# Seven products, then six mixing tiles: another order of work in a mixture-of-experts stage

## The chip, the cores and the metric

The kernel runs on one core of one Trainium2 chip. The core has TensorE (PE in the views; its weight loads are shown apart as PEld), VectorE (DVE), ScalarE (ACT), GpSimd (POOL) and SyncE (SP), which run their own instruction streams and meet only at semaphores. The metric is the device time of one execution in microseconds (us).

## The reference, cut to what matters

Local attention with a few global positions makes x (1536 tokens, 512 wide). Then follow a mixture of experts and a gated layer:

```python
def _moe_ref(x, domain_probs, w1, w2):
    p = domain_probs / (domain_probs.sum(-1, keepdims=True) + 1e-09)
    out = np.zeros((N, D))
    for e in range(E):                       # 4 experts, hidden width 1024
        h = np.maximum(x @ w1[e], 0.0)
        out += p[:, e:e + 1] * (h @ w2[e])
    return out

def _moe2_ref(x, w_in, w_out, g_ln):
    h = x @ w_in
    ...                                      # softmax gate, layer norm
    return ln @ w_out
```

## The kernel before

**Steps.** The experts are worked in 32 steps, numbered s = 0 to 31. A step takes a group of 256 hidden columns (16 groups g) for one half of the tokens. Every fp32 operand is split in a high and a low part, and each product of two matrices is three matmuls (high by high, high by low, low by high). x @ w1 is done as a 2 by 2 block product with seven products in place of eight (Strassen-Winograd), in the order 1, 2, 6, 7, 5, 4, 3: `product(s, n)`, six matmuls of 128x384 each, 42 in a step. h @ w2 is done in six token tiles: `mix(s, t)`, six matmuls of 128x512 each, 36 in a step. TensorE mixes step s-1 while it makes the products of step s. Steps 4 to 27 are a hardware loop of four steps a turn; the others are written out.

**What follows the products.** The seven products share four PSUM banks and the mixing tiles three. ScalarE copies product 1 to `kept` (`keep`, L1211). VectorE adds up the products in seven additions that count `p_sum`: `first_block`, `second_sum`, `third_sum`, `last_block`, `fourth_sum`, `lower_block`, `right_block` (L1549 to L1577). Each reads a PSUM bank. Four of them finish a block of h. ScalarE then writes relu of that block as the high part (`relu_hi`, L1216) and VectorE the low part (`relu_lo`, L1582, both inputs in SBUF, counts `h_split`). `add_up(s, t)` (L1598) adds a mixed tile times its expert weight to `acc` and frees the tile's PSUM bank.

**Waits of TensorE that matter here.** Product 5 waits for `keep`, product 4 for `first_block`, product 3 for `second_sum` of its own step, since they reuse the banks; mix t of a step waits for `add_up` t-3.

**GpSimd** prepares the weights with operations that read and write SBUF alone: `weigh_sums` and `weigh_parts` split a group of w1 and start when all products of step 2g-3 are there; `split_w2` starts when all tiles of step 2g-3 are mixed. After the last group, SyncE loads w_in, and GpSimd makes four block sums of it (128x1024 each, L770 to L777, once w_in is there and the products of step 29 are) and then seven low parts (`win_lo_at`, L783, each after ScalarE's high part `win_hi_part`, L1356). ScalarE's order in steps 30 and 31 is written out by hand.

**The tail** (from L1028 and L1104 on) turns `acc`, multiplies by w_in and w_out and writes the output.

Of the kernel before, what the change touches and what calls it, by code (L numbers as in the profile page):

```python
# [23 lines left out]
START = 16  # L24
# [29 lines left out]
def attention_experts_solu_kernel(nc, H, qkW, qT, kT, v, counts_in, probs, w1, w2, w_in, w_out, gain, out):  # L54
# [16 lines left out]
    TILES = QB  # L71
# [31 lines left out]
    with ExitStack() as base:  # L103
# [740 lines left out]
        def _(pe):  # L844

            def product(s, n, i, g, slot, bt):

                bank = p_bank(i, n)
                if n == 1:
                    pe.wait_ge(w1_ready, g + 1)  # L850
                    at_least(pe, p_sum, SETS * s - 4)
                if n == 2:
                    at_least(pe, p_sum, SETS * s - 2)
                if n == 6:
                    at_least(pe, p_sum, SETS * s - 1)
                if n == 7:
                    at_least(pe, p_sum, SETS * s)
                if n == 5:
                    pe.wait_ge(p_kept, s + 1)
                if n == 4:  # L860
                    pe.wait_ge(p_sum, SETS * s + 1)
                if n == 3:
                    pe.wait_ge(p_sum, SETS * s + 2)
                part = {1: 0, 2: 1, 4: 2, 3: 3, 5: 4, 6: 5, 7: 6}[n]
                for kk in range(2):
                    for w, x in ((1, 1), (1, 0), (0, 1)):
                        mm = nc.tensor.matmul(bank, ws[slot][:, w, part, kk, :], xs[:, 2 * bt + kk, x, part, :],  # L867
                                              start=(kk == 0 and w == 1 and x == 1),
                                              stop=(kk == 1 and w == 0))
                mm.then_inc(p_done, 1)  # L870

            def mix(s, t, slot, ring, g):

                if t == 0:
                    pe.wait_ge(w2_ready, g + 1)
                    pe.wait_ge(h_split, BLOCKS * s + 3)
                if t == 3:
                    pe.wait_ge(h_split, BLOCKS * s + BLOCKS)
                if isinstance(s, int) and s == LAST and t == 5:
                    pe.wait_ge(x2_raw, 6)  # L880
                else:
                    at_least(pe, acc_written, TILES * s + t + 1 - Y_BANKS + (isinstance(s, int) and s == LAST and t == 4))
                tok = slice((t % 3) * P, (t % 3 + 1) * P)
                for f in range(2):
                    b = 2 * f + t // 3
                    for h, w in ((1, 1), (1, 0), (0, 1)):
                        mm = nc.tensor.matmul(mixed_at(s, t), hs[ring][:, h, b, tok], w2s[slot][:, w, f, :],  # L887
                                              start=(f == 0 and h == 1 and w == 1), stop=(f == 1 and h == 0))
                mm.then_inc(y_done, 1)
# [128 lines left out]
            def turn_x(s):  # L1018
# [9 lines left out]
                    mm = nc.tensor.transpose(turned_at(s)[:, k * P:(k + 1) * P], acc[:, s, k * P:(k + 1) * P], ident[:, :])  # L1028
                mm.then_inc(x_final, 1)

            def step(a, i):

                s, g, last = 4 * a + i, group(a, i), 4 * a + i - 1
                slot, bt, ring = slot_of(a, i), batch(a, i), (i - 1) % 2
                last_slot, last_g = (slot_of(a, i - 1), group(a, i - 1)) if i else (1, 2 * a - 1)
                new = isinstance(a, int) and s == 1
                if new:
                    pe.wait_ge(xs_sum, START + 21)
                product(s, 1, i, g, slot, bt)
                product(s, 2, i, g, slot, bt)  # L1040
                mix(last, 0, last_slot, ring, last_g)
                mix(last, 1, last_slot, ring, last_g)
                if new:
                    pe.wait_ge(xs_sum, START + 24)
                mix(last, 2, last_slot, ring, last_g)
                if new:
                    pe.wait_ge(xs_lo, START + 13)
                product(s, 6, i, g, slot, bt)
                if new:
                    pe.wait_ge(xs_lo, START + 14)  # L1050
                product(s, 7, i, g, slot, bt)
                mix(last, 3, last_slot, ring, last_g)
                if new:
                    pe.wait_ge(xs_lo, START + 15)
                product(s, 5, i, g, slot, bt)
                mix(last, 4, last_slot, ring, last_g)
                if new:
                    pe.wait_ge(xs_lo, START + 16)
                product(s, 4, i, g, slot, bt)
                if isinstance(a, int) and s == LAST:  # L1060
                    turn_x(0)
                    turn_x(1)
                product(s, 3, i, g, slot, bt)
                mix(last, 5, last_slot, ring, last_g)

            for i in range(1, 4):
                step(0, i)
# [126 lines left out]
        def _(act):  # L1194
# [12 lines left out]
            def keep(s, i):  # L1207

                act.wait_ge(p_done, SETS * s + 1)
                at_least(act, p_sum, SETS * s - 5)  # L1210
                nc.scalar.activation(kept[:, 0, :], p_bank(i, 1), ACT.Copy).then_inc(p_kept, 1)  # L1211

            def relu_hi(s, b, bt):

                act.wait_ge(p_sum, SETS * s + {0: 1, 3: 4, 2: 6, 1: 7}[b])
                nc.scalar.activation(hs[bt][:, 1, b], hs_sum[bt][:, 0, b], ACT.Relu).then_inc(hhi_ready, 1)  # L1216
# [151 lines left out]
                for c in chunks:  # L1368
                    wout_hi_part(c)

            keep(LAST - 1, 2)
            relu_hi(LAST - 1, 0, 0)
            act.wait_ge(win_loaded, 16)
            act.wait_ge(p_done, SETS * (LAST - 1))
            for at in range(3):
# [126 lines left out]
        def _(dve):  # L1502
# [294 lines left out]
            with dve.Else():  # L1797
                attend_wide()

            def halve(a, i):  # L1800

                s, bt = 4 * a + i, i % 2
                first = isinstance(a, int) and s <= 2
                expert = a // 2 if i else (a - 1) // 2
                last_bt = batch(a, i - 1) if i else 1
                first_block(s, i)
                add_up(s - 1, 0, last_bt, expert, first)
                relu_lo(s, 0, bt)
                add_up(s - 1, 1, last_bt, expert, first)
                add_up(s - 1, 2, last_bt, expert, first)  # L1810
                second_sum(s, i)
                third_sum(s, i)
                add_up(s - 1, 3, last_bt, expert, first)
                last_block(s, i)
                fourth_sum(s, i)
                add_up(s - 1, 4, last_bt, expert, first)
                relu_lo(s, 3, bt)
                lower_block(s, i)
                right_block(s, i)
                relu_lo(s, 2, bt)  # L1820
                relu_lo(s, 1, bt)
                add_up(s - 1, 5, last_bt, expert, first)

            for i in range(1, 4):
                halve(0, i)
# [224 lines left out]
```

## Time and profile before

| what | value |
|---|---|
| median of 3 runs | 741.29 us (740.76 to 741.61) |
| the profiled execution's own time | 741.24 us |
| its span in the trace | 739.2 us |
| PE busy | 734.8 us (99% of the span) |
| DVE, ACT, POOL busy | 516.6, 223.5, 348.1 us |
| granted clock of TensorE | full speed in all 40 slices |

The time of an execution is about 2 us more than its span. Busy PE is pipelined matmuls, so that a start-to-start distance tells more than a busy time: a 128x512 matmul is shown as 0.39 us long, but the next one starts after 0.23 us.

### The profile page before, as it was taken

To read this page: it belongs to the slowest core of one execution; us is meant where nothing else is said; L and a number is where in the kernel's file an instruction comes from. 1 tells how busy PE (TensorE), PEld (TensorE's weight loads), DVE (VectorE), ACT (ScalarE), POOL (GpSimd) and SP (SyncE) were. 2 spreads that over 40 slices of the span, in tenths; PEclk is the share of its full clock that TensorE was granted. 3 is DMA by queue.
4 is the path that set the end of the run, shared out by engine and by line. 5 is a ranking of instruction groups with operands and counts; after the bars stand their busy time and mean duration, and the time that the engine had idled before them with its cause. 6 is when DMAs were issued, how large, how long until landed. Compare 5 with 4: busy or idle time off the path is not lost.

```text
span 739.2 us, 12549 instructions
## 1 busy us (share of the span) xinstructions
PE 734.8 (99%) x3992; PEld 650.0 (88%) x3992; DVE 516.6 (70%) x1031; ACT 223.5 (30%) x421; POOL 348.1 (47%) x336
## 2 busy tenths in 40 slices
PE   9999999999999999999999999999999999999998
PEld 7888899999898998899998989989998888888887
DVE  5777767676666766767666676766668858767773
ACT  5667741111111121111111111111115466433332
POOL 4558446253542536435264351644519986432400
PEclk9999999999999999999999999999999999999999
DMA  8835300100101000010000101000030300000001
GB/s 227 241 109 147 106 31 1 58 29 30 33 25 57 28 28 28 28 57 28 28 28 28 57 8 48 28 28 0 0 114 5 110 1 11 19 30 28 15 30 43
DMA packets 38226, 36.11 MB, mean 49 GB/s; under 512 B 14512, under 2 KB 31152, under 8 KB 38192
## 3 DMA queue, kind: packets, MB, share of 16 engines
q1 hardware_dynamic: 36448, 33.46, 14.3%
q10 hardware_dynamic: 1744, 2.23, 0.9%
q8 instruction: 17, 0.28, 0.2%
q14 instruction: 17, 0.14, 0.1%
HBM read 32.54 MB, written 3.15 MB: 48 GB/s over the span
## 4 chain that ended last, share of the span: by engine, by line
PE 97%; DVE 2%; DMA 1%; issue 0%; SPq 0%; ACT 0%; POOL 0%; DVEq 0%
PE y_ps L887 35%; PE p_ps L867 32%; PE o_ps L934 5%; PE pT_ps L915 3%; PE s_ps L905 3%; PE up_ps L1106 3%; PE up_ps L1104 3%; PE up_ps L1105 3%; PE out_ps L1134 2%; PE out_ps L1136 2%; PE out_ps L1135 2%; PE lnT_ps L1119 1%; PE xt_ps L945 1%; PE xr_ps L1028 1%; DMA qk<-in_qkW 1%
## 5 line engine op out<-in xcount | busy, mean ns | idle before, releaser
L887 PE MATMUL y_ps<-w2s,hs 128*128 128x512 f32 x1140 | 283.0, 393 | 0.2 <-DVE acc L1598 0.2
L867 PE MATMUL p_ps<-xs,ws 128*128 128x384 f32 x1344 | 254.9, 335 | 0.0
L867 PEld LDWEIGHTS p_ps<-xs,ws 128*128 128x128 f32 x1344 | 237.5, 188 | 10.7
L887 PEld LDWEIGHTS y_ps<-w2s,hs 128*128 128x128 f32 x1140 | 211.8, 188 | 38.9 <-DVE acc L1598 0.8
L1598 DVE SCALAR_TENSOR_TENSOR acc<-y_ps,pr,acc 128x512 f32<-128x512 f32 x178 | 132.9, 748 | 77.0 <-PE y_ps L887 76.3
L1216 ACT ACTIVATE hs<-hs_sum 128x384 fp32r<-128x384 f32 x128 | 67.2, 525 | 350.2 <-DVE hs_sum L1563 231.6
L1582 DVE SCALAR_TENSOR_TENSOR hs<-hs_sum,hs 128x384 fp32r<-128x384 f32 x128 | 97.4, 771 | 4.3 <-ACT hs L1216 2.3
L648 POOL TENSOR_TENSOR ws_sum<-raw_sum 128x256 f32<-128x256 f32 x16 | 11.8, 741 | 148.8 <-PE p_ps L867 144.6
L679 POOL CAST w2s<-raw_sum 128x1024 fp32r<-128x1024 f32 x16 | 16.9, 1056 | 84.9 <-PE y_ps L887 84.9
L1229 ACT ACTIVATE neg_s<-neg_s,row 128x256 f32<-128x256 f32 (+1 forms) x96 | 41.9, 482 | 27.1 <-DVE row L1620 26.9
L1620 DVE CUSTOM_DVE_ANT_0 neg_s<-s_ps,bias 128x256 f32<-128x256 f32 (+1 forms) x87 | 31.2, 398 | 15.9 <-PE s_ps L905 13.2
L934 PE MATMUL o_ps<-v_sb,pT 128*128 128x65 f32 x352 | 42.3, 272 | 0.0
L934 PEld LDWEIGHTS o_ps<-v_sb,pT 128*128 128x128 f32 x352 | 41.2, 192 | 0.7 <-DVE x_pair L1646 0.7
L682 POOL TENSOR_TENSOR w2s<-raw_sum,w2s 128x1024 fp32r<-128x1024 f32 x16 | 38.4, 2400 | 2.9 <-POOL w2s L679 2.9
L671 POOL TENSOR_TENSOR ws<-ws_sum,ws 128x1024 fp32r<-128x1024 f32 x16 | 38.4, 2398 | 2.9 <-POOL ws L668 2.9
L824 POOL TENSOR_TENSOR stats<-stats,minus_half 128x1 f32<-128x1 f32 x12 | 10.3, 854 | 59.0 <-DVE stats L1918 59.0
L1549 DVE TENSOR_TENSOR hs_sum<-p_ps,kept 128x384 f32<-128x384 f32 x32 | 17.8, 557 | 26.7 <-PE p_ps L867 26.4
L1104 PE MATMUL up_ps<-win_hi,x 128*128 128x512 f32 x84 | 34.1, 406 | 0.0
L1106 PE MATMUL up_ps<-win_hi,x 128*128 128x512 f32 x84 | 32.9, 392 | 0.0
L1135 PE MATMUL out_ps<-wout_lo_a,ln_hi 128*128 128x512 f32 x77 | 30.0, 389 | 0.0
L1211 ACT ACTIVATE kept<-p_ps 128x384 f32<-128x384 f32 x32 | 15.8, 492 | 42.0 <-PE p_ps L867 42.0
L1558 DVE TENSOR_TENSOR kept<-p_ps,kept 128x384 f32<-128x384 f32 x32 | 17.8, 557 | 13.9 <-PE p_ps L867 13.5
(200 smaller groups left out, 976.0 us busy)
## 6 DMA issues: line engine op xcount, KB each, us to landing
raw_sum<-in_w SPq DMA_DIRECT2D x28, 512.0 KB, 3.3
qk<-in_qkW SPq DMA_DIRECT2D x16, 256.0 KB, 3.3
qk<-in_qkW SPq DMA_DIRECT2D x31, 128.0 KB, 3.4
v_sb<-in_v SPq DMA_DIRECT2D x16, 192.0 KB, 3.2
out<-o_sb SPq DMA_DIRECT2D x11, 256.0 KB, 2.0
raw_sum<-in_w ACTq DMA_DIRECT2D x4, 512.0 KB, 6.6
raw_sum<-in_w_in SPq DMA_DIRECT2D x1, 2048.0 KB, 7.6
wout_lo_a_sum<-in_w_out SPq DMA_DIRECT2D x1, 1792.0 KB, 7.6
```

The lines of the kernel that those rows point to most:

```text
L671: nc.gpsimd.tensor_tensor(lo[:, 3:7], sum_[:, 3:7], f32(hi[:, 3:7]), ALU.subtract).then_inc(w1_ready, 1)
L682: nc.gpsimd.tensor_tensor(lo, rows, f32(hi), ALU.subtract).then_inc(w2_ready, 1)
L867: mm = nc.tensor.matmul(bank, ws[slot][:, w, part, kk, :], xs[:, 2 * bt + kk, x, part, :], start=(kk == 0 and w == 1 and x == 1), stop=(kk ...
L887: mm = nc.tensor.matmul(mixed_at(s, t), hs[ring][:, h, b, tok], w2s[slot][:, w, f, :], start=(f == 0 and h == 1 and w == 1), stop=(f == 1 ...
L934: mm = nc.tensor.matmul(o_ps[:, m, i * DV:(i + 1) * DV], pT[c % 2][:, e, (2 * m + half) * P:(2 * m + half + 1) * P], v_sb[:, p, m, at, :], ...
L1104: nc.tensor.matmul(up_bank(q, n), x_hi, win_hi[:, part, kk], start=(kk == 0), stop=False)
L1106: mm = nc.tensor.matmul(up_bank(q, n), x_lo, win_hi[:, part, kk], start=False, stop=(kk == KH - 1))
L1135: nc.tensor.matmul(out_ps[m][:, :], ln_hi[m][:, c, :], wout_lo(c), start=False, stop=False)
L1216: nc.scalar.activation(hs[bt][:, 1, b], hs_sum[bt][:, 0, b], ACT.Relu).then_inc(hhi_ready, 1)
L1229: nc.scalar.activation(tile, tile, ACT.Exp, bias=row[:, b // STEPS_PAIR, m, i:i + 1], scale=-1.0).then_inc(exp_ready, 1)
L1582: nc.vector.scalar_tensor_tensor(hs[bt][:, 0, b], hs_sum[bt][:, 0, b], 0.0, f32(hs[bt][:, 1, b]), ALU.max, ALU.subtract).then_inc(h_split, 1)
L1598: nc.vector.scalar_tensor_tensor(acc[:, tile, :], mixed_at(s, t), weight, acc[:, tile, :], ALU.mult, ALU.add).then_inc(acc_written, 1)
```

## The change

TensorE's `step` now makes all seven products of the step and then mixes all six tiles of the last step. Step 1, whose products wait for the attention stage, keeps the old order in a function of its own (`first_step`; the waits for `xs_sum` and `xs_lo` are only there). VectorE's `halve` follows: the additions and low parts come first, `add_up` of tile 0 is put before the low part of block 1, and the other five `add_up` come after it; step 1 keeps its order (`first_halve`). ScalarE makes the first five high parts of w_in before it starts step 30, and the last two before the `relu_hi` of block 3. No instruction is added or removed.

```diff
             def step(a, i):
...
                 if new:
                     pe.wait_ge(xs_sum, START + 21)
+                    first_step(s, i, g, slot, bt, ring, last, last_slot, last_g)
+                    return
                 product(s, 1, i, g, slot, bt)
                 product(s, 2, i, g, slot, bt)
-                mix(last, 0, last_slot, ring, last_g)
-                mix(last, 1, last_slot, ring, last_g)
...
-                mix(last, 2, last_slot, ring, last_g)
...
                 product(s, 6, i, g, slot, bt)
...
                 product(s, 7, i, g, slot, bt)
-                mix(last, 3, last_slot, ring, last_g)
...
                 product(s, 5, i, g, slot, bt)
-                mix(last, 4, last_slot, ring, last_g)
...
                 product(s, 4, i, g, slot, bt)
                 if isinstance(a, int) and s == LAST:
                     turn_x(0)
                     turn_x(1)
                 product(s, 3, i, g, slot, bt)
-                mix(last, 5, last_slot, ring, last_g)
+                for t in range(TILES):
+                    mix(last, t, last_slot, ring, last_g)
...
-            keep(LAST - 1, 2)
-            relu_hi(LAST - 1, 0, 0)
             act.wait_ge(win_loaded, 16)
             act.wait_ge(p_done, SETS * (LAST - 1))
             for at in range(3):
...
             for at in range(3, 5):
                 win_hi_part(at)
-            relu_hi(LAST - 1, 3, 0)
+            keep(LAST - 1, 2)
+            relu_hi(LAST - 1, 0, 0)
             act.wait_ge(win_sum, 4)
             for at in range(5, SETS):
                 win_hi_part(at)
+            relu_hi(LAST - 1, 3, 0)
             relu_hi(LAST - 1, 2, 0)
             relu_hi(LAST - 1, 1, 0)
...
+                first_block(s, i)
+                relu_lo(s, 0, bt)
+                second_sum(s, i)
+                third_sum(s, i)
+                last_block(s, i)
+                fourth_sum(s, i)
+                relu_lo(s, 3, bt)
+                lower_block(s, i)
+                right_block(s, i)
+                relu_lo(s, 2, bt)
+                add_up(s - 1, 0, last_bt, expert, first)
+                relu_lo(s, 1, bt)
+                for t in range(1, TILES):
+                    add_up(s - 1, t, last_bt, expert, first)
```

TensorE, one of the steps 28 to 30, before (L867 is a product's matmul, L887 a mixing tile's):

```order
L867 MATMUL p_ps<-xs,ws 128x384 x12
L887 MATMUL y_ps<-w2s,hs 128x512 x18
L867 MATMUL p_ps<-xs,ws 128x384 x12
L887 MATMUL y_ps<-w2s,hs 128x512 x6
L867 MATMUL p_ps<-xs,ws 128x384 x6
L887 MATMUL y_ps<-w2s,hs 128x512 x6
L867 MATMUL p_ps<-xs,ws 128x384 x12
L887 MATMUL y_ps<-w2s,hs 128x512 x6
```

and steps 28 to 30 with the change:

```order
L867 MATMUL p_ps<-xs,ws 128x384 x42
L887 MATMUL y_ps<-w2s,hs 128x512 x36
L867 MATMUL p_ps<-xs,ws 128x384 x42
L887 MATMUL y_ps<-w2s,hs 128x512 x36
L867 MATMUL p_ps<-xs,ws 128x384 x42
L887 MATMUL y_ps<-w2s,hs 128x512 x36
```

Eight changes between the two kinds of matmul in a step have become two.

VectorE, the start of step 30 before (L1549 is `first_block`, L1598 `add_up`, L1582 `relu_lo`):

```order
L1549 TENSOR_TENSOR hs0_sum<-p_ps3,kept 128x384
L1598 SCALAR_TENSOR_TENSOR acc<-y_ps0,pr,acc 128x512
L1582 SCALAR_TENSOR_TENSOR hs0<-hs0_sum,hs0 128x384
L1598 SCALAR_TENSOR_TENSOR acc<-y_ps1,pr,acc 128x512
L1598 SCALAR_TENSOR_TENSOR acc<-y_ps2,pr,acc 128x512
L1553 TENSOR_TENSOR kept<-p_ps0,kept 128x384
L1558 TENSOR_TENSOR kept<-p_ps1,kept 128x384
L1598 SCALAR_TENSOR_TENSOR acc<-y_ps0,pr,acc 128x512
L1563 TENSOR_TENSOR hs0_sum<-p_ps2,kept 128x384
L1566 TENSOR_TENSOR hs0_sum<-p_ps2,kept 128x384
L1598 SCALAR_TENSOR_TENSOR acc<-y_ps1,pr,acc 128x512
L1582 SCALAR_TENSOR_TENSOR hs0<-hs0_sum,hs0 128x384
```

and with the change (L1558 is now `first_block`, L1607 `add_up`, L1591 `relu_lo`):

```order
L1558 TENSOR_TENSOR hs0_sum<-p_ps3,kept 128x384
L1591 SCALAR_TENSOR_TENSOR hs0<-hs0_sum,hs0 128x384
L1562 TENSOR_TENSOR kept<-p_ps0,kept 128x384
L1567 TENSOR_TENSOR kept<-p_ps1,kept 128x384
L1572 TENSOR_TENSOR hs0_sum<-p_ps2,kept 128x384
L1575 TENSOR_TENSOR hs0_sum<-p_ps2,kept 128x384
L1591 SCALAR_TENSOR_TENSOR hs0<-hs0_sum,hs0 128x384
L1586 TENSOR_TENSOR hs0_sum<-p_ps3,kept 128x384
L1580 TENSOR_TENSOR hs0_sum<-p_ps0,hs0_sum 128x384
L1591 SCALAR_TENSOR_TENSOR hs0<-hs0_sum,hs0 128x384
L1607 SCALAR_TENSOR_TENSOR acc<-y_ps0,pr,acc 128x512
L1591 SCALAR_TENSOR_TENSOR hs0<-hs0_sum,hs0 128x384
```

Three of the four `relu_lo` of a step now stand ahead of its first `add_up`.

ScalarE around step 30 with the change (L1220 is `keep`, L1225 `relu_hi`, L1365 `win_hi_part`; before, the first group of five high parts stood behind the `keep` and `relu_hi` that now follow it, and the other two behind a further `relu_hi`):

```order
L1365 ACTIVATE win_hi<-raw_sum 128x1024 x3
L1365 ACTIVATE win_hi<-t_lo_sum 128x1024 x2
L1220 ACTIVATE kept<-p_ps 128x384
L1225 ACTIVATE hs<-hs_sum 128x384
L1365 ACTIVATE win_hi<-t_lo_sum 128x1024
L1365 ACTIVATE win_hi<-raw_sum 128x1024
L1225 ACTIVATE hs<-hs_sum 128x384 x3
```

The copy of product 1 of step 30 now stands behind five operations on w_in. GpSimd's and SyncE's own orders stay as they were.

## Rows read from the trace of the kernel before

**Rows 1.** The page: the chain that ended last, by engine.

```profile
PE 97%; DVE 2%; DMA 1%; issue 0%; SPq 0%; ACT 0%; POOL 0%; DVEq 0%
```

**Rows 2.** Timeline of PE, one step: start us, us, instruction [idle before].

```profile
172.66 2.27 PE L867 MATMUL p_ps<-xs,ws 128*128 128x384 f32 x12
174.77 1.55 PE L887 MATMUL y_ps<-w2s,hs 128*128 128x512 f32 x6
176.16 1.21 PE L867 MATMUL p_ps<-xs,ws 128*128 128x384 f32 x6
177.20 1.55 PE L887 MATMUL y_ps<-w2s,hs 128*128 128x512 f32 x6
...
184.15 4.28 PE L887 MATMUL y_ps<-w2s,hs 128*128 128x512 f32 x18
188.27 2.27 PE L867 MATMUL p_ps<-xs,ws 128*128 128x384 f32 x12
```

**Rows 3.** Timeline of PE cut inside a row of 18 mixing matmuls.

```profile
248.66 2.20 PE L887 MATMUL y_ps<-w2s,hs 128*128 128x512 f32 x9
250.70 2.27 PE L867 MATMUL p_ps<-xs,ws 128*128 128x384 f32 x12
```

**Rows 4.** Timeline of PE, steps 30 and 31 begin.

```profile
556.62 2.25 PE L867 MATMUL p_ps<-xs,ws 128*128 128x384 f32 x12
...
561.78 1.67 PE L887 MATMUL y_ps<-w2s,hs 128*128 128x512 f32 x6 [0.15 <-DVE acc L1598]
...
572.67 2.25 PE L867 MATMUL p_ps<-xs,ws 128*128 128x384 f32 x12
```

**Rows 5.** Timeline of DVE, from step 29 to step 31.

```profile
554.02 0.55 DVE L1582 SCALAR_TENSOR_TENSOR hs<-hs_sum,hs 128x384 fp32r<-128x384 f32 x1
554.48 0.55 DVE L1577 TENSOR_TENSOR hs_sum<-p_ps,kept 128x384 f32<-128x384 f32 x1
...
555.91 5.16 DVE L1582 SCALAR_TENSOR_TENSOR hs<-hs_sum,hs 128x384 fp32r<-128x384 f32 x2
560.99 0.74 DVE L1598 SCALAR_TENSOR_TENSOR acc<-y_ps,pr,acc 128x512 f32<-128x512 f32 x1
...
580.70 0.54 DVE L1553 TENSOR_TENSOR kept<-p_ps,kept 128x384 f32<-128x384 f32 x1
581.35 0.56 DVE L1558 TENSOR_TENSOR kept<-p_ps,kept 128x384 f32<-128x384 f32 x1
```

**Rows 6.** Timeline of POOL in the same stretch.

```profile
542.62 2.40 POOL L682 TENSOR_TENSOR w2s<-raw_sum,w2s 128x1024 fp32r<-128x1024 f32 x1 [0.18 <-POOL w2s L679]
555.57 2.40 POOL L770 TENSOR_TENSOR t_lo_sum<-raw_sum 128x1024 f32<-128x1024 f32 x1 [10.55 <-PE p_ps L867]
557.91 2.73 POOL L771 TENSOR_TENSOR t_lo_sum<-raw_sum 128x1024 f32<-128x1024 f32 x1
560.61 2.71 POOL L774 TENSOR_TENSOR t_lo_sum<-raw_sum,t_lo_sum 128x1024 f32<-128x1024 f32 x1
563.50 2.51 POOL L777 TENSOR_TENSOR raw_sum<-raw_sum,t_lo_sum 128x1024 f32<-128x1024 f32 x1 [0.18 <-POOL t_lo_sum L774]
566.22 7.47 POOL L783 TENSOR_TENSOR raw<-raw_sum,win_hi 128x1024 fp32r<-128x1024 f32 x3 [0.20 <-POOL raw_sum L777]
```

**Rows 7.** Timeline of ACT in the same stretch.

```profile
555.07 0.53 ACT L1216 ACTIVATE hs<-hs_sum 128x384 fp32r<-128x384 f32 x1 [1.99 <-DVE hs_sum L1577]
...
557.87 0.49 ACT L1211 ACTIVATE kept<-p_ps 128x384 f32<-128x384 f32 x1 [1.32 <-PE p_ps L867]
...
562.65 2.95 ACT L1356 ACTIVATE win_hi<-raw_sum 128x1024 fp32r<-128x1024 f32 x3
```

**Rows 8.** The page: DMA issues, KB each, us to landing.

```profile
raw_sum<-in_w_in SPq DMA_DIRECT2D x1, 2048.0 KB, 7.6
```

**Rows 9.** Timeline of PE: step 2 begins.

```profile
119.64 2.25 PE L867 MATMUL p_ps<-xs,ws 128*128 128x384 f32 x12
```

**Rows 10.** Timeline of POOL: the last operation on w1 of group 2.

```profile
127.20 2.42 POOL L671 TENSOR_TENSOR ws<-ws_sum,ws 128x1024 fp32r<-128x1024 f32 x1 [0.18 <-POOL ws L668]
```

More of the change, by code:

```diff
@@ L1029, in turn_x, with first_step @@
                 mm.then_inc(x_final, 1)
+            def first_step(s, i, g, slot, bt, ring, last, last_slot, last_g):
+                product(s, 1, i, g, slot, bt)
+                product(s, 2, i, g, slot, bt)
+                mix(last, 0, last_slot, ring, last_g)
+                mix(last, 1, last_slot, ring, last_g)
+                pe.wait_ge(xs_sum, START + 24)
+                mix(last, 2, last_slot, ring, last_g)
+                pe.wait_ge(xs_lo, START + 13)
+                product(s, 6, i, g, slot, bt)
+                pe.wait_ge(xs_lo, START + 14)
+                product(s, 7, i, g, slot, bt)
+                mix(last, 3, last_slot, ring, last_g)
+                pe.wait_ge(xs_lo, START + 15)
+                product(s, 5, i, g, slot, bt)
+                mix(last, 4, last_slot, ring, last_g)
+                pe.wait_ge(xs_lo, START + 16)
+                product(s, 4, i, g, slot, bt)
+                product(s, 3, i, g, slot, bt)
+                mix(last, 5, last_slot, ring, last_g)
             def step(a, i):
@@ L1038, in step @@
                     pe.wait_ge(xs_sum, START + 21)
+                    first_step(s, i, g, slot, bt, ring, last, last_slot, last_g)
+                    return
                 product(s, 1, i, g, slot, bt)
                 product(s, 2, i, g, slot, bt)
-                mix(last, 0, last_slot, ring, last_g)
-                mix(last, 1, last_slot, ring, last_g)
-                if new:
-                    pe.wait_ge(xs_sum, START + 24)
-                mix(last, 2, last_slot, ring, last_g)
-                if new:
-                    pe.wait_ge(xs_lo, START + 13)
                 product(s, 6, i, g, slot, bt)
-                if new:
-                    pe.wait_ge(xs_lo, START + 14)
                 product(s, 7, i, g, slot, bt)
-                mix(last, 3, last_slot, ring, last_g)
-                if new:
-                    pe.wait_ge(xs_lo, START + 15)
                 product(s, 5, i, g, slot, bt)
-                mix(last, 4, last_slot, ring, last_g)
-                if new:
-                    pe.wait_ge(xs_lo, START + 16)
                 product(s, 4, i, g, slot, bt)
@@ L1798, in _, with first_halve @@
                 attend_wide()
[L1800 to L1805, printed above, removed]
+            def first_halve(s, i, bt, last_bt, expert, first):
                 first_block(s, i)
@@ L1822, in halve @@
                 add_up(s - 1, 5, last_bt, expert, first)
+            def halve(a, i):
+                s, bt = 4 * a + i, i % 2
+                first = isinstance(a, int) and s <= 2
+                expert = a // 2 if i else (a - 1) // 2
+                last_bt = batch(a, i - 1) if i else 1
+                if isinstance(a, int) and s == 1:
+                    first_halve(s, i, bt, last_bt, expert, first)
+                    return
+                first_block(s, i)
[12 more added lines that the diff above has]
+                    add_up(s - 1, t, last_bt, expert, first)
             for i in range(1, 4):
```

## The prediction

> **What bounds the kernel now.** I read the chain that ended last first. It is TensorE for 97% of the span [rows 1], so that only what changes the distance between TensorE's own matmuls, or makes it wait, moves the time. Then I read TensorE's timeline over one ordinary step and wrote down where each block of matmuls starts. The step lasts 188.27 - 172.66 = 15.61 us [rows 2], and the same pattern comes back in every step of the loop with no idle time. Then I asked what lies in those 15.61 us beside the matmuls' own pace. Six products' matmuls take 177.20 - 176.16 = 1.04 us, or 0.1733 us each [rows 2]; the last nine of 18 mixing matmuls take 250.70 - 248.66 = 2.04 us, or 0.2267 us each [rows 3]. By these paces a step is 42 x 0.1733 + 36 x 0.2267 = 7.28 + 8.16 = 15.44 us. The missing 0.17 us is at the changes from one kind to the other: six mixing matmuls behind a product take 176.16 - 174.77 = 1.39 us and not 1.36, 18 take 4.12 and not 4.08, and the 12 product matmuls behind them 2.11 and not 2.08 [rows 2]. Last I looked at the only place in the expert steps where TensorE is idle, step 30, and at what VectorE, GpSimd and ScalarE do there. The reader is to see that VectorE's two low parts (L1582), which take 0.55 us when GpSimd is quiet, take 5.16 us for the pair there [rows 5], and that they end at 561.07, just when GpSimd's operation from 557.91 ends (560.64) plus one low part [rows 6]. GpSimd in turn takes 2.34 us from start to start when VectorE did not push in (555.57 to 557.91) and 2.70 when it did (557.91 to 560.61). So a low part waits for the end of the GpSimd operation in progress, goes in between two, and puts GpSimd back by 0.35 us. Additions that read PSUM show no such wait.
>
> **Term 1, fewer changes.** With two changes a step the excess is one long mixing block, 4.12 - 4.08 = 0.04, and one product block behind a long mixing block, 2.11 - 2.08 = 0.03 us. That is 0.07 in place of 0.17, or 0.10 us less in each of the steps 2 to 31: **-3.0 us**. Bounds: 0 (if the excess belongs to the tile and not to the change) and -5.1 (all 0.17 in 30 steps). I take the value of the rows that have the very sequence.
>
> The Trainium skill, "TensorE: Matmul & The Clock Gate", section "Wait — 56ns, not 53.3ns?", gives back-to-back matmuls their columns at 2.4 GHz plus a fixed 2.5 ns, without regard to the order. An estimate by that page is 42 x 0.1625 + 36 x 0.2158 = 14.6 us a step, which this trace doesn't bear out (15.61), and it makes this term 0.
>
> **Term 2, the ordinary steps' waits.** I laid the new order of a step on its clock, 0 being its first matmul. Products end at 1.05, 2.11, then every 1.04 to 7.31; tiles end at 8.7, 10.1, 11.4, 12.8, 14.2, 15.5. VectorE sees a product 0.2 us after its end (as ScalarE does: 557.87 against 556.62 + 1.04 [rows 4, 7]). The second sum is ready near 5.0 and product 3 wants it at 6.27. `add_up` 0 is done at 9.7, and tile 3 wants it at 11.4; `add_up` 1 at 11.0, tile 4 wants it at 12.8. So each has 1.3 us or more of cover. GpSimd's w1 work now starts at 7.7 and not at 14 in its step: there its operations are 0.4 to 1.3 us long, and its 2.4 us one falls at 1.5 to 3.8 of the next step, ahead of the low part at 3.5. **0 us**; if the cover is gone, each stall is some 0.3 us in one step of two.
>
> Step 2 is the exception. Step 1 keeps its order, so GpSimd's w1 work there keeps its time, and its long operation starts 127.20 - 119.64 = 7.6 us into step 2 [rows 9, 10], before the low part of block 2 (9.0) or before that of block 1 (9.6). In the first case `add_up` 0 is done near 12.5 and tile 3 is 1.1 us late; in the second `add_up` 1 is 0.35 us late. The two are a few hundredths of a us apart: **+0.5 us**, bounds 0.3 and 1.2.
>
> **Term 3, the stall that goes.** Step 30 lasts 572.67 - 556.62 = 16.05 us, 0.44 more than an ordinary step: tile 2 waited for an `add_up` that stood behind the 5.16 us pair [rows 4, 5]. In the new order tile 2 asks for an `add_up` of the step before: **-0.44 us**.
>
> **Term 4, step 30.** The last split of w2 ends at 542.62 + 2.40 = 545.02 [rows 6] and w_in lands 7.6 us later [rows 8], at 552.6, which is 11.6 us into step 29 (it began at 556.62 - 15.61 = 541.0). Both don't move against the step. Before, GpSimd then had to wait for the step's last product (555.57); now the products are done at 7.3, so it starts at 11.8. Its four sums follow each other at 2.35 us with a 0.2 gap ahead of the fourth [rows 6]: the second ends at 16.5, the fourth at 21.4. A step is now 15.5 us: these are 1.0 and 5.9 in step 30.
>
> ScalarE makes three high parts, waits for the second sum until 1.0, and makes two more (2.95 us for three, [rows 7]) until 3.0. Only then comes `keep` (0.49), 2 us later than its input. `first_block` 0.56 and `relu_hi` 0.53 follow: the low part of block 0 is ready at 4.7 and has to wait for the fourth sum's end, E = 5.9. From E on I count with the rows' distances: a low part ahead to the next instruction 0.39 (561.07 - 560.99 off 0.47), sum to dependent sum 0.65 [rows 5], sum to ScalarE 0.59 (554.48 to 555.07, [rows 5, 7]), ScalarE to VectorE 0.56, GpSimd's seven low parts of w_in without a gap, 2.35 each or 2.70 with a low part let in.
>
> - `second_sum` E+0.39, done E+1.0 = 6.9. Product 3 wanted it at 6.27 and starts 0.65 late; tile 0 starts at E+2.1, tile 3 would at E+6.2.
> - `third_sum` E+1.04, `last_block` E+1.69, `relu_hi` E+2.28: the low part of block 3 is ready at E+2.84. GpSimd's boundary was at E+2.70. It is missed by 0.14 and the next is at E+5.05.
> - `lower_block` E+5.44, `relu_hi` E+6.03, low part of block 2 ready E+6.6, boundary E+7.75. `add_up` 0 at E+8.14, done E+8.9: tile 3 is 2.7 us late.
> - Low part of block 1: boundary E+10.45; `add_up` 1 done E+11.6. Tile 4 would have started at E+10.3: 1.3 us late.
> - Two more tiles: the step ends at E+14.4 = 20.3, not 15.5. **+4.8 us.** `keep` itself delays no one; what costs is four low parts in a chain, each behind a 2.35 us operation, ahead of the `add_up`s.
>
> In step 31 GpSimd's seventh operation ends at about 3.4 us, when the first low part is ready, and its next ones are half as long (they read 512 columns): `add_up` 0 near 11.2, wanted at 12.3. 0 us there and in the tail, which has the same order.
>
> **Sum.** -3.0 + 0.5 - 0.44 + 4.8 = +1.9 us on the profiled execution's 741.24: **743.1 us**. The median of the runs is 741.29, 0.05 us from it. Bounds of this case by its own terms: step 2 between 0.3 and 1.2, step 30 by 0.5 either way: 742.3 to 744.4.
>
> **The rivals.**
> - *A caught boundary.* If the low part of block 3 is ready 0.14 us sooner against GpSimd, it goes in at E+2.7, block 2 at E+5.4, and `add_up` 0 is done at E+6.6, 0.3 late; block 1 at E+8.1 makes tile 4 1.4 us late. Step 30 then costs 2.4 and the time is 740.7. For it: 0.14 us is little. Against it: both sides hang on the same instant E, so that the margin doesn't drift.
> - *The low parts slip through (the other side).* GpSimd's hold costs less than a whole operation, for it waits for high parts from a late ScalarE, or a low part finds it in a gap. The place is step 30, and the change is faster than before as soon as that step loses under 2.9 us; with nothing lost there and 0.3 in step 2 it gives 741.24 - 3.44 + 0.3 = 738.1. For it: single low parts of that stretch waited 0.4 us only. Against it: the 5.16 us pair. The Trainium skill, "SBUF — State Buffer", section "SBUF: two separate sides", has the loser block for the other's whole instruction when a VectorE operation has two SBUF inputs; by that rule, the trace agrees, this rival gets little.
> - *The changes were not the cost.* The excess stays at 0.17 a step, because it belongs to each tile's first matmuls: -0.44 + 0.5 + 4.8 gives 746.1. Against it: the first six of an 18 block must carry all of the block's 0.04, the second and third tile in it nothing [rows 2, 3]. It is here that the skill's fixed cost per matmul would end.
> - *Stalls in ordinary steps.* Low parts behind GpSimd's w1 work, now in the middle of a step, make tile 4 wait 0.3 us in 14 steps: 4.2 us more, 747.
>
> **How the numbers follow.** The forecast 0.50, the caught boundary 0.16, slipping through 0.18, changes without cost 0.09, ordinary stalls 0.07. This kernel's measurement tells about 0.2% (1.5 us) from no change, so faster is under 739.8 and slower over 742.8. Slower: three quarters of the forecast's own spread and the last two rivals, 0.53. Same: the rest of the forecast and most of the caught boundary, 0.26. Faster: 0.21. The range 739.6 to 744.9 leaves out most of the slipping case and the two dear rivals.
>
> **What would show it.** Right: an ordinary step of 15.51 us start to start with two block changes; in step 30 a `keep` near 3.0 us, product 3 about 0.7 late, tile 3 and tile 4 waiting for VectorE's `acc` by 2.7 and 1.3 us, low parts of over 2 us under L1591 there; step 30 about 20 us long; steps 29 and 31 without a wait. Wrong: a step still of 15.6 us, or a PE without idle in step 30, or waits for `acc` in the loop.

## The result, and the profile after

| what | before | after |
|---|---|---|
| median of 15 runs each | 741.21 us (740.76 to 741.92) | 742.65 us (742.37 to 745.23) |
| ratio after : before | | 1.0023 [1.0016, 1.0030] |
| the profiled execution's own time | 741.24 us | 742.49 us |
| its span | 739.2 us | 740.4 us |
| PE, DVE busy | 734.8, 516.6 us | 732.4, 511.0 us |

The kernel became 1.4 us slower. That is small, but it is the difference of two much larger amounts. The page of the changed kernel, the chain that ended last by engine:

```profile
PE 93%; DVE 3%; DMA 1%; POOL 1%; issue 1%; ACT 1%; ACTq 0%; DVEq 0%; POOLq 0%; SPq 0%
```

TensorE was 97% of it [rows 1]. Everything else now has about 7%. The waits of PE in the changed kernel (us in total, times, longest) name VectorE twice:

```profile
PE y_ps L887 <- DVE acc L1607: 3.4, 2, 2.5
...
PE p_ps L867 <- DVE kept L1562: 0.8, 1, 0.8
```

The two lines hold three waits, 4.2 us. The timeline of PE in the changed kernel shows first an ordinary step, then the mixing of step 29 and step 30:

```profile
196.95 7.47 PE L867 MATMUL p_ps<-xs,ws 128*128 128x384 f32 x42
204.25 8.36 PE L887 MATMUL y_ps<-w2s,hs 128*128 128x512 f32 x36
212.45 7.47 PE L867 MATMUL p_ps<-xs,ws 128*128 128x384 f32 x42
...
545.40 8.36 PE L887 MATMUL y_ps<-w2s,hs 128*128 128x512 f32 x36
553.60 6.43 PE L867 MATMUL p_ps<-xs,ws 128*128 128x384 f32 x36
560.81 1.33 PE L867 MATMUL p_ps<-xs,ws 128*128 128x384 f32 x6 [0.78 <-DVE kept L1562]
561.97 4.28 PE L887 MATMUL y_ps<-w2s,hs 128*128 128x512 f32 x18
568.76 1.63 PE L887 MATMUL y_ps<-w2s,hs 128*128 128x512 f32 x6 [2.51 <-DVE acc L1607]
571.32 3.02 PE L887 MATMUL y_ps<-w2s,hs 128*128 128x512 f32 x12 [0.93 <-DVE acc L1607]
574.18 6.43 PE L867 MATMUL p_ps<-xs,ws 128*128 128x384 f32 x36
```

These rows answer to [rows 2] and [rows 4]. An ordinary step takes 212.45 - 196.95 = 15.50 us in place of 15.61. Step 30 takes 574.18 - 553.60 = 20.58 us in place of 16.05. All three waits of PE lie in step 30: product 3 waits 0.78 us for `second_sum`, tile 3 2.51 us for `add_up` 0, and tile 4 0.93 us for `add_up` 1.

What VectorE did in that step (changed kernel, timeline of DVE; L1591 is `relu_lo`, L1607 `add_up`) answers to [rows 5]:

```profile
557.42 0.56 DVE L1558 TENSOR_TENSOR hs_sum<-p_ps,kept 128x384 f32<-128x384 f32 x1 [2.87 <-ACT kept L1220]
558.58 1.71 DVE L1591 SCALAR_TENSOR_TENSOR hs<-hs_sum,hs 128x384 fp32r<-128x384 f32 x1 [0.59 <-ACT hs L1225]
...
562.67 2.64 DVE L1591 SCALAR_TENSOR_TENSOR hs<-hs_sum,hs 128x384 fp32r<-128x384 f32 x1
...
566.37 1.59 DVE L1591 SCALAR_TENSOR_TENSOR hs<-hs_sum,hs 128x384 fp32r<-128x384 f32 x1
567.88 0.74 DVE L1607 SCALAR_TENSOR_TENSOR acc<-y_ps,pr,acc 128x512 f32<-128x512 f32 x1
568.54 2.07 DVE L1591 SCALAR_TENSOR_TENSOR hs<-hs_sum,hs 128x384 fp32r<-128x384 f32 x1
```

and GpSimd beside it (changed kernel, timeline of POOL), which answers to [rows 6]:

```profile
550.15 2.41 POOL L770 TENSOR_TENSOR t_lo_sum<-raw_sum 128x1024 f32<-128x1024 f32 x1 [8.07 <-DMA raw_sum<-in_w_in]
...
557.46 2.41 POOL L777 TENSOR_TENSOR raw_sum<-raw_sum,t_lo_sum 128x1024 f32<-128x1024 f32 x1 [0.18 <-POOL t_lo_sum L774]
560.07 7.47 POOL L783 TENSOR_TENSOR raw<-raw_sum,win_hi 128x1024 fp32r<-128x1024 f32 x3 [0.20 <-POOL raw_sum L777]
567.50 7.71 POOL L783 TENSOR_TENSOR t_lo<-t_lo_sum,win_hi 128x1024 fp32r<-128x1024 f32 x3
```

The same view, cut so that the second and the third of those operations stand alone:

```profile
562.51 2.38 POOL L783 TENSOR_TENSOR raw<-raw_sum,win_hi 128x1024 fp32r<-128x1024 f32 x1
564.86 2.68 POOL L783 TENSOR_TENSOR raw<-raw_sum,win_hi 128x1024 fp32r<-128x1024 f32 x1
```

Two things are to be seen. First, GpSimd's first block sum now follows the landing of w_in, where it followed a product before. Second, the low parts of VectorE end 0.42 to 0.46 us, a little less than one quiet low part (0.55), after GpSimd has ended an operation or gone on to the next: at 558.58 + 1.71 = 560.29 (GpSimd's fourth sum ended at 557.46 + 2.41 = 559.87), at 562.67 + 2.64 = 565.31 (GpSimd's next began at 564.86) and at 566.37 + 1.59 = 567.96 (567.50). The four take 8.0 us together, where four quiet ones would take 2.2. The `add_up` between them, whose tile is read from PSUM, takes its usual 0.74 us, although GpSimd is busy all through it.

### The profile page after: what moved, and what is told of

Read it like the earlier page. It is cut to its first block, busy times and chain, and to the rows that moved or that the text cites. A ratio compares the mean times of both kernels' runs of the same rounds, so it can differ in the third digit from the quotient of the medians.

```text
span 740.4 us, 12549 instructions
## 1 busy us (share of the span) xinstructions
PE 732.4 (99%) x3992; PEld 650.3 (88%) x3992; DVE 511.0 (69%) x1031; ACT 221.6 (30%) x421; POOL 340.9 (46%) x336
## 4 chain that ended last, share of the span: by engine, by line
PE 93%; DVE 3%; DMA 1%; POOL 1%; issue 1%; ACT 1%; ACTq 0%; DVEq 0%; POOLq 0%; SPq 0%
PE y_ps L887 33%; PE p_ps L867 30%; PE o_ps L934 5%; PE pT_ps L915 3%; PE s_ps L905 3%; PE up_ps L1115 3%; PE up_ps L1113 3%; PE up_ps L1114 3%; PE out_ps L1143 2%; PE out_ps L1145 2%; PE out_ps L1144 2%; PE lnT_ps L1128 1%; DMA raw_sum<-in_w_in 1%; PE xt_ps L945 1%; PE xr_ps L1028 1%
## 5 line engine op out<-in xcount | busy, mean ns | idle before, releaser
L887 PE MATMUL y_ps<-w2s,hs 128*128 128x512 f32 x1140 | 265.9, 390 | 3.4 <-DVE acc L1607 3.4
L887 PEld LDWEIGHTS y_ps<-w2s,hs 128*128 128x128 f32 x1140 | 213.3, 188 | 47.5 <-DVE hs L1591 2.9
L867 PE MATMUL p_ps<-xs,ws 128*128 128x384 f32 x1344 | 240.4, 335 | 0.8 <-DVE kept L1562 0.8
L867 PEld LDWEIGHTS p_ps<-xs,ws 128*128 128x128 f32 x1344 | 234.5, 188 | 3.7 <-DVE kept L1562 1.1
L1607 DVE SCALAR_TENSOR_TENSOR acc<-y_ps,pr,acc 128x512 f32<-128x512 f32 x178 | 133.1, 749 | 73.3 <-PE y_ps L887 72.5
L1225 ACT ACTIVATE hs<-hs_sum 128x384 fp32r<-128x384 f32 x128 | 65.5, 526 | 156.2 <-DVE hs_sum L1572 78.7
L1591 DVE SCALAR_TENSOR_TENSOR hs<-hs_sum,hs 128x384 fp32r<-128x384 f32 x128 | 91.0, 712 | 28.2 <-ACT hs L1225 20.5
L1220 ACT ACTIVATE kept<-p_ps 128x384 f32<-128x384 f32 x32 | 15.7, 492 | 229.3 <-PE p_ps L867 229.3
L1558 DVE TENSOR_TENSOR hs_sum<-p_ps,kept 128x384 f32<-128x384 f32 x32 | 17.9, 558 | 44.3 <-PE p_ps L867 41.2
L915 PEld LDWEIGHTS pT_ps<-ident,neg_s 128*128 128x128 f32 x176 | 18.9, 141 | 8.3 <-issue 5.1
```

Source lines behind the costliest of these rows:

```text
L915: mm = nc.tensor.transpose(pT_ps[e][:, (2 * m + half) * P:(2 * m + half + 1) * P], neg_s[:, slot_of_tile(b, e, m), half * P:(half + 1) * P ...
L1591: nc.vector.scalar_tensor_tensor(hs[bt][:, 0, b], hs_sum[bt][:, 0, b], 0.0, f32(hs[bt][:, 1, b]), ALU.max, ALU.subtract).then_inc(h_split, 1)
L1607: nc.vector.scalar_tensor_tensor(acc[:, tile, :], mixed_at(s, t), weight, acc[:, tile, :], ALU.mult, ALU.add).then_inc(acc_written, 1)
```

## The experiments

All are edits of the changed kernel. The kernel before, run on the same chips, had medians of 741.26 us and, for the experiments on the last two steps alone, on GpSimd held back and on four changes, 741.25 us.

### Steps 30 and 31 in the old order

```diff
             def step(a, i):
...
+                if isinstance(a, int) and s >= LAST - 1:
+                    ...                      # products and tiles in the order before
+                    return
...
-                if isinstance(a, int) and s == 1:
+                if isinstance(a, int) and s == 1 or (isinstance(a, int) and s >= LAST - 1):
                     first_halve(s, i, bt, last_bt, expert, first)
```

ScalarE's order for the last steps is the one before, too. This leaves the gain of the steps 2 to 29 alone.

> Steps 2 to 29 in the new order, steps 30 and 31 and ScalarE's last two steps as before the change. If the loss of 20.59 - 15.61 = 5 us belongs to step 30 alone (the forecast's theory), it goes and the 0.10 us a step stays: step 30 near 15.6 us without an idle TensorE, since the low parts of step 29 are now out of the way before GpSimd starts on w_in, and some 4.6 us less than the changed kernel, 738.0. If the loss were a matter of the new order anywhere near w_in's work (a rival: the stall moves to step 29 or 31), 741 or more.

Measured: 737.92 us, ratio to the kernel before 0.9957 [0.9943, 0.9971]. TensorE's timeline of this kernel around step 30:

```profile
554.45 2.27 PE L867 MATMUL p_ps<-xs,ws 128*128 128x384 f32 x12
...
570.07 2.25 PE L867 MATMUL p_ps<-xs,ws 128*128 128x384 f32 x12
```

Step 30 is 570.07 - 554.45 = 15.62 us, without a wait; even the 0.44 us of before are gone. The gain of 3.3 us by the medians is these 0.44 and 28 steps in the new order (2.8 us), and the new kernel's loss is all in its last two steps.

### The new order in the last two steps alone

The reverse: steps 2 to 29 as before, steps 30 and 31 as in the change.

```diff
+                if not isinstance(a, int) or 1 < s < LAST - 1:
+                    ...                      # products and tiles in the order before
+                    return
...
-                if isinstance(a, int) and s == 1:
+                if isinstance(a, int) and s == 1 or (not isinstance(a, int) or 1 < s < LAST - 1):
                     first_halve(s, i, bt, last_bt, expert, first)
```

> Steps 2 to 29 as before the change, steps 30 and 31 and ScalarE's last steps as in the change. Theory: none of the 0.10 us a step is saved (ordinary steps 15.61), and step 30 loses more than in the changed kernel, for in the old order step 29 leaves its products late, and GpSimd starts on w_in 3 us later against the step, so that the fourth sum and with it the low parts come later: product 5, product 3 and tiles 3 and 4 wait, step 30 near 23.7 us and the time near 748.7. Rival (the loss of step 30 is fixed, whatever stands ahead): step 30 at 20.6, 745.8.

Measured: 748.38 us, ratio 1.0108 [1.0080, 1.0135], the dearest of all. TensorE's timeline of this kernel in step 30:

```profile
556.47 4.33 PE L867 MATMUL p_ps<-xs,ws 128*128 128x384 f32 x24
562.96 2.38 PE L867 MATMUL p_ps<-xs,ws 128*128 128x384 f32 x12 [2.17 <-ACT kept L1237]
566.63 1.31 PE L867 MATMUL p_ps<-xs,ws 128*128 128x384 f32 x6 [1.29 <-DVE kept L1579]
...
574.60 6.07 PE L887 MATMUL y_ps<-w2s,hs 128*128 128x512 f32 x18 [2.53 <-DVE acc L1624]
580.50 6.43 PE L867 MATMUL p_ps<-xs,ws 128*128 128x384 f32 x36
```

Step 30 is 24.03 us. With step 29 in the old order, GpSimd's sums start only behind its last product (555.41), the last two of ScalarE's five high parts behind the second sum, and `keep` behind those, so that product 5 waits as well (2.17 us). In the change, the new order of step 29 lets GpSimd begin 550.15 - 545.40 = 4.8 us into the mixing, and so softens what the new order of step 30 costs.

Part of the 24.03 us is another thing. Here is PE by stretches in this kernel (from:to, length and busy us, matmuls, granted clock, DMA share, GB/s):

```profile
574.00:574.50 0.50, 0.00 (x0) 1.00 1.05 410
577.00:578.00 1.00, 1.00 (x3) 0.50 0.00 0
579.00:580.00 1.00, 1.00 (x6) 1.00 0.00 0
```

Behind waits of 2.17, 1.29 and 2.53 us within one step, TensorE's granted clock was half, 1.2 in place of 2.4 GHz, from about 575.0 to 578.2 us. Tile 3 took 2.54 us (574.60 to 577.14) and not 1.36. From tile 3 to the end of the step it is 580.50 - 574.60 = 5.90 us, against 574.18 - 568.76 = 5.42 in the change, so that the low clock cost about 0.5 us net: it also covered the wait of tile 4. The expectation of 23.7 us for this step did not have this term.

### ScalarE's order as before

```diff
+            keep(LAST - 1, 2)
+            relu_hi(LAST - 1, 0, 0)
             act.wait_ge(win_loaded, 16)
...
-            keep(LAST - 1, 2)
-            relu_hi(LAST - 1, 0, 0)
+            relu_hi(LAST - 1, 3, 0)
...
-            relu_hi(LAST - 1, 3, 0)
```

This puts ScalarE's order back: `keep` and the first `relu_hi` stand ahead of the five high parts again, and the `relu_hi` of block 3 ahead of the last two. Nothing else is changed.

> The changed kernel with ScalarE's order of before in step 30 (the copy of product 1 and the first high part ahead of the five operations on w_in). Theory (GpSimd's long operations hold off VectorE's low parts): only product 3's wait of 0.8 us goes and the first of the four low parts gets in earlier, waits for acc stay at tiles 3 and 4; step 30 near 18 us, part of it given back in step 31; about 741.4. Rival (ScalarE's copy behind five high parts is the cause): nearly all of 5 us comes back, 738.

Measured: 741.16 us, ratio 1.0000 [0.9991, 1.0009]. Timeline of PE in step 30 of this kernel:

```profile
553.53 7.47 PE L867 MATMUL p_ps<-xs,ws 128*128 128x384 f32 x42
...
566.35 1.62 PE L887 MATMUL y_ps<-w2s,hs 128*128 128x512 f32 x6 [1.24 <-DVE acc L1607]
568.91 3.03 PE L887 MATMUL y_ps<-w2s,hs 128*128 128x512 f32 x12 [0.94 <-DVE acc L1607]
571.78 6.43 PE L867 MATMUL p_ps<-xs,ws 128*128 128x384 f32 x36
```

With the early `keep` the first low part starts at 556.98, gets in ahead of GpSimd's fourth sum (from 557.32) and takes 0.57 us, and product 3 no longer waits. Step 30 is 18.25 us: 2.3 us better, not whole. The other low parts still stand ahead of the `add_up`s. A new wait of 0.56 us in step 31, for a sum behind a low part of 2.69 us, gives some of it back. The rival, that ScalarE's late copy is the whole cause, would have brought nearly 5 us.

### GpSimd's low parts in four pieces

```diff
-                nc.gpsimd.tensor_tensor(win_lo_at(n), win_sum_at(n), f32(win_hi[:, n]), ALU.subtract
-                                        ).then_inc(winlo_ready, 1)
+                for piece in range(4):
+                    ...                      # the same subtraction on 256 of the 1024 columns
+                low.then_inc(winlo_ready, 1)
```

The work is the same, but none of the seven low parts of w_in can hold VectorE for longer than one piece. The four sums ahead of them stay whole.

> The changed kernel; each of GpSimd's seven low parts of w_in is done as four operations of 256 columns in place of one of 1024, the same work in shorter holds. Theory of the hold: a low part of VectorE waits 0.7 us at most, the waits of tiles 3 and 4 go, product 3's stays (it comes from the fourth block sum, left whole); step 30 near 16.2 us, about 738.5. Rival (VectorE simply reaches add_up 0 too late in the new order, or GpSimd and VectorE share a rate and the total counts): step 30 stays near 20 us, 742.6.

Measured: 738.58 us, ratio 0.9965 [0.9953, 0.9977]. DVE in this kernel (L1594 is `relu_lo`), and the GpSimd pieces beside it:

```profile
558.61 1.70 DVE L1594 SCALAR_TENSOR_TENSOR hs<-hs_sum,hs 128x384 fp32r<-128x384 f32 x1 [0.59 <-ACT hs L1228]
...
562.70 0.72 DVE L1594 SCALAR_TENSOR_TENSOR hs<-hs_sum,hs 128x384 fp32r<-128x384 f32 x1
...
564.48 0.66 DVE L1594 SCALAR_TENSOR_TENSOR hs<-hs_sum,hs 128x384 fp32r<-128x384 f32 x1
565.06 0.74 DVE L1610 SCALAR_TENSOR_TENSOR acc<-y_ps,pr,acc 128x512 f32<-128x512 f32 x1
```

```profile
560.11 9.43 POOL L785 TENSOR_TENSOR raw<-raw_sum,win_hi 128x256 fp32r<-128x256 f32 x12 [0.20 <-POOL raw_sum L777]
```

No order changed, only the length of GpSimd's operations, and the low parts fell from 2.64, 1.59 and 2.07 us to 0.72, 0.66 and 1.13. The first one, held by a whole sum, kept its 1.70, and product 3 still waits (0.60 us). `add_up` is never late, although three low parts of w_in now take GpSimd 9.4 us in place of 7.4. This shows that the length of GpSimd's single operation, not its total work, sets the price.

### GpSimd's low parts held back

```diff
             pool.wait_ge(win_sum, 4)
+            pool.wait_ge(h_split, BLOCKS * (LAST - 1) + BLOCKS)
             for i, n in enumerate(WIN_ORDER):
                 pool.wait_ge(winhi_ready, i + 1)
```

GpSimd starts its seven low parts only when the four low parts of step 30 are done.

> The changed kernel; GpSimd starts its seven low parts of w_in only when VectorE has finished the four low parts of step 30. Theory: tiles 3 and 4 of step 30 wait no more (product 3's 0.8 us stays), step 30 near 16.2 us; but the seven operations now run through step 31, so its low parts are held off there: a wait of a turn and of tile 3 there, near 2 us together. In all about 740.8. Rival (GpSimd's operations don't matter): 742.6, with the waits in step 30 as they were.

Measured: 740.86 us, ratio 0.9995 [0.9986, 1.0005]. In step 30 of this kernel the last three low parts take 0.56 us each, tiles 3 and 4 don't wait, product 3 does (0.94 us), and the step is 570.53 - 553.79 = 16.74 us. The hold comes back one step later; its timelines of PE and POOL:

```profile
570.53 6.43 PE L868 MATMUL p_ps<-xs,ws 128*128 128x384 f32 x36
...
577.67 0.63 PE L1029 MATMUL up_ps<-ident,acc 128*128 128x128 f32 x4 [0.27 <-DVE kept L1568]
...
584.91 5.38 PE L888 MATMUL y_ps<-w2s,hs 128*128 128x512 f32 x22 [1.44 <-DVE acc L1608]
```

```profile
566.50 7.13 POOL L784 TENSOR_TENSOR raw<-raw_sum,win_hi 128x1024 fp32r<-128x1024 f32 x3 [6.28 <-DVE hs L1592]
```

The two engines' waits move with their overlap: where they don't meet, no low part is long; where they do, they are (2.41 and 2.64 us in step 31). That is why this kernel as a whole is no faster than the one before.

### VectorE's low parts between the `add_up`s

```diff
+                if isinstance(a, int) and s >= LAST - 1:
+                    ...                      # the seven additions of products
+                    add_up(s - 1, 0, last_bt, expert, first)
+                    relu_lo(s, 0, bt)
+                    add_up(s - 1, 1, last_bt, expert, first)
+                    add_up(s - 1, 2, last_bt, expert, first)
+                    relu_lo(s, 3, bt)
+                    add_up(s - 1, 3, last_bt, expert, first)
+                    relu_lo(s, 2, bt)
+                    add_up(s - 1, 4, last_bt, expert, first)
+                    relu_lo(s, 1, bt)
+                    add_up(s - 1, 5, last_bt, expert, first)
+                    return
```

TensorE keeps the new order in all steps, and GpSimd its long operations. Only what stands behind a held low part is changed.

> The changed kernel; in steps 30 and 31 VectorE does all seven additions first and puts the four low parts between the add_ups (low part of block 0 after add_up 0, of 3 after 2, of 2 after 3, of 1 after 4). TensorE and ScalarE as in the change. Theory: what hurt was the chain of four held low parts ahead of the add_ups, so neither product 3 nor tiles 3 and 4 wait: step 30 at 15.5 us, 4.8 us less than the changed kernel, 737.8. Rival (ScalarE's late copy): product 3 and tiles still wait, over 741.

Measured: 737.50 us, ratio 0.9949 [0.9935, 0.9962], the lowest median of the study (the first experiment's 737.92 lies within its interval) and below both kernels. DVE in this kernel:

```profile
562.65 0.75 DVE L1607 SCALAR_TENSOR_TENSOR acc<-y_ps,pr,acc 128x512 f32<-128x512 f32 x1 [0.83 <-PE y_ps L887]
563.32 2.04 DVE L1591 SCALAR_TENSOR_TENSOR hs<-hs_sum,hs 128x384 fp32r<-128x384 f32 x1
```

The low parts are as slow as ever (2.04, 1.43, 2.09 and 2.09 us), and PE has no wait in step 30, which takes 15.51 us. So their length costs only where they stand ahead of the sums and the `add_up`s. The kernel in four pieces shows the same from the other side: in the same place, short ones cost little.

### Four changes a step in place of two

```diff
                 product(s, 7, i, g, slot, bt)
+                for t in range(3):
+                    mix(last, t, last_slot, ring, last_g)
                 product(s, 5, i, g, slot, bt)
...
-                for t in range(TILES):
+                for t in range(3, TILES):
                     mix(last, t, last_slot, ring, last_g)
```

VectorE's order follows; steps 30 and 31 are as before.

> As the run with the last two steps in the old order, but steps 2 to 29 with four changes a step: products 1, 2, 6, 7, tiles 0 to 2, products 5, 4, 3, tiles 3 to 5. If the excess is 0.04 us for a row of mixing matmuls behind products and 0.026 for products behind a long row of them, a step has 0.134 over the 15.44 of its own paces: 15.57 us, 0.066 more than with two changes, 28 times 1.85: 739.8. Rival (0.17 us in eight changes is 0.021 each, so four changes are 0.085): 15.53, 738.4.

Measured: 740.69 us, ratio 0.9990 [0.9980, 1.0000]. One step of this kernel on PE, and the starts of steps 30 and 31:

```profile
540.74 4.35 PE L867 MATMUL p_ps<-xs,ws 128*128 128x384 f32 x24
544.92 4.28 PE L887 MATMUL y_ps<-w2s,hs 128*128 128x512 f32 x18
549.04 3.31 PE L867 MATMUL p_ps<-xs,ws 128*128 128x384 f32 x18
552.19 4.28 PE L887 MATMUL y_ps<-w2s,hs 128*128 128x512 f32 x18
556.31 2.27 PE L867 MATMUL p_ps<-xs,ws 128*128 128x384 f32 x12
558.94 4.35 PE L887 MATMUL y_ps<-w2s,hs 128*128 128x512 f32 x18 [0.36 <-DVE acc L1623]
...
572.52 2.25 PE L867 MATMUL p_ps<-xs,ws 128*128 128x384 f32 x12
```

A step is 556.31 - 540.74 = 15.57 us, the number expected. The excess over the 15.44 us of pure pace is thus 0.17, 0.13 and 0.07 us with eight, four and two changes. An equal price per change would have given 15.53 us for four. What does fit is a price for each pair of a long mixing row and the product row behind it (0.04 + 0.03 us), of which this step has two and the new one one. The total missed the expectation by 0.9 us. Step 30 is 572.52 - 556.31 = 16.21 us here, 0.59 more than the 15.62 of the first experiment, for the wait shown in it, which the argument had overlooked: the pair of low parts of step 29 comes late here as it did before [rows 5]. The profiled executions of the two kernels both begin step 2 at 120.28 us and end 2.4 us apart by their spans, which is 28 x 0.067 and these 0.59. The medians are 2.8 apart; the other 0.3 us are within the interval of 0.1%. The pair took 5.05 us in this kernel, 5.16 before.

## Why the prediction was right

The time came out at 742.65 against the forecast 743.1 us, through the mechanism forecast.

**Term 1 was right.** From the start of step 2 to that of step 30 the time fell from 556.62 - 119.64 = 436.98 us [rows 4, 9] to 553.60 - 119.43 = 434.17, by 2.81 us in 28 steps: 0.10 a step, as in the text. So the rival that the changes were not the cost falls, and with it the bound of -5.1: three kernels with 8, 4 and 2 changes have steps of 15.61, 15.57 and 15.50 us. For the kernel, the fixed price per matmul of the Trainium skill, "TensorE: Matmul & The Clock Gate", section "Wait — 56ns, not 53.3ns?", would leave the three alike; they aren't.

**Term 2 was right for the ordinary steps and wrong for step 2.** PE has no wait in the steps 3 to 29, so the stalls in ordinary steps didn't come. The text had GpSimd's place wrong there, without harm: the 2.4 us operation on w1 starts 0.1 us into the next step (212.55) and not 1.5; at 1.6 us (198.52) it is the one on w2, and in step 29 that one held the first low part to 0.95 us (541.55), which the text did not have. For step 2 the text gave +0.5 us; measured was 134.92 - 119.43 = 15.49 us, nothing. Here are GpSimd and VectorE in the changed kernel there:

```profile
126.75 2.52 POOL L671 TENSOR_TENSOR ws<-ws_sum,ws 128x1024 fp32r<-128x1024 f32 x1 [0.18 <-POOL ws L668]
```

```profile
128.06 1.62 DVE L1591 SCALAR_TENSOR_TENSOR hs<-hs_sum,hs 128x384 fp32r<-128x384 f32 x1
129.61 0.74 DVE L1604 TENSOR_SCALAR acc<-y_ps,pr 128x512 f32<-128x512 f32 x1
```

GpSimd's operation starts 7.3 us into the step (7.6 in the text), and it does hold the low part of block 2, which takes 1.62 us. The step that failed is "`add_up` 0 is done near 12.5": an operation that runs from 7.6 to 10.0 lets the low part end at 10.4 and `add_up` 0 at 11.2, within the 11.4 at which tile 3 wants it. It was mis-added (12.5 would need the operation to start near 9.0), and the trace has 129.61 + 0.74 - 119.43 = 10.9. The second case has the same slip: a low part of block 1 held by the same operation would also end near 10.4, and `add_up` 1 near 11.2, long before the 12.8 of tile 4.

**Term 3 was right.** No tile 2 waits in step 30, in the change or in the kernels with the old order there. (In the kernel with four changes it is tile 0 that waits.)

**Term 4 was right in kind and in size.** Step 30 lost 20.58 - 15.50 = 5.08 us against an ordinary new step, where the text had 4.8, and each link is in the rows (E is the end of the fourth sum):

| step of the argument | text | trace |
|---|---|---|
| fourth sum ends, into the step | 5.9 | 559.87 - 553.60 = 6.3 |
| `keep` starts | 3.0 | 3.3 |
| product 3 waits | 0.65 | 0.78 |
| low part of block 3 is ready after E | 2.84 | 562.67 - 559.87 = 2.80 |
| GpSimd's boundary after E | 2.70, missed by 0.14 | 562.51 - 559.87 = 2.64, missed by 0.16 |
| `add_up` 0 starts after E | 8.14 | 8.01 |
| tile 3 waits | 2.7 | 2.51 |
| tile 4 waits | 1.3 | 0.93 |

So the boundary was missed by as little as forecast, and the rival of the caught boundary falls, though narrowly. The rival of the low parts that slip through falls by the four low parts of 1.71, 2.64, 1.59 and 2.07 us (the text looked for low parts of over 2 us: two of the four were). The two experiments that take away the hold (four pieces) or the overlap (held back) show the cause; the one with the low parts between the `add_up`s shows the path. That VectorE's operation with both inputs in SBUF is blocked for the whole of a GpSimd instruction that reads SBUF and started first is what the Trainium skill, "SBUF — State Buffer", section "SBUF: two separate sides", says; these traces agree, and the price fell with the length of GpSimd's instruction.

**One sentence of term 4 was too strong.** "`keep` itself delays no one": with an early `keep` step 30 is 18.25 us and not 20.58. It delayed no one directly, but it brought the first low part into GpSimd's fourth sum (558.58, the sum runs from 557.46) and not ahead of it (556.98 with the early `keep`), and 2.3 us hung on that.

**The sum.** From one profiled execution to the other: steps 2 to 29 -2.81; step 30 +4.53; step 31 to the last turn of `acc` -0.27 (0.13 of it a small stall there that also went); ahead of step 2 and in the tail -0.25, which no part of the change explains. Together +1.2 us, where the text had +1.9: the 0.5 of step 2 is most of the difference. The 0.13 and the 0.25, which the text did not foresee, go the same way, and the 0.28 us that step 30 cost beyond the text goes the other, so that a part of the closeness is luck: errors that stand against each other. Two smaller things: the text's own bounds add up to 742.4 to 744.3, a tenth off what it gives, and by its own line (slower is over 742.8) the 742.65 us fall on the side "same", to which it gave 0.26, and not on "slower" with 0.53.

**What the text did not have at all: TensorE's clock.** In 10 of the 15 executions of the changed kernel the mean granted clock was 0.998 or 0.995, and these took 742.43 to 745.23 us. The other five had 1.0 and 742.37 to 742.58. The kernel before had 1.0 in all 36 executions beside the experiments, and so had every kernel of the experiments but the one with the new order in the last two steps alone, whose four executions had 0.998 or 0.995. These two are the kernels in which TensorE waits 2.5 us at once. In the latter's trace the low clock lies right behind the waits of step 30. For the changed kernel only an execution with 1.0 was traced, so that the same place is likely there, but not shown.

## What to carry to other kernels

Before an order is made coarser to save small costs at each change of work, look at what each engine's queue holds between a wait and its release: here 0.10 us in each of 28 steps was paid back in a single step, because low parts that another engine can hold for up to 2.1 us each came to stand ahead of the operations that free PSUM. Put operations that can be held behind those that free a buffer, or cut the holder's instruction in pieces; either gave nearly the whole gain (737.5 and 738.6 us), and a loop's exit needs its order worked out by itself.

## What the runs showed of the hardware

- A row of 36 mixing matmuls takes 8.20 us, only 0.04 more than 36 x 0.2267, the same excess as a row of 18 has (4.12 against 4.08, [rows 2, 3]). The first half of a row carries it: the last nine of 18 are the very rows that gave the 0.2267. Why the first are slower was not tried.
- GpSimd's subtraction costs 2.36 us for 1024 columns (three from 566.50 to 573.58 in the kernel with the low parts held back), and twelve pieces of 256 took 9.43 us, 0.79 each with VectorE's low parts let in, or 3.1 for 1024. GpSimd's added time was hidden here.
- VectorE's operation with one input in PSUM (`add_up`, 0.74 us) kept its length beside a busy GpSimd, in every kernel.
- A stall can cost more than its length: behind 6.0 us of waits in one step TensorE's granted clock was 0.50 for about 3.2 us (the kernel with the new order in the last two steps alone). The kernel with GpSimd's low parts held back, whose longest wait there was 1.44 us, had 1.0 in all ten executions.
